# Attention stage of a three-stage kernel: the output product in two halves, with a reordered load and store queue

## The chip, the core and the metric

The program runs on one core of a Trainium2 chip. The metric is the time of one execution on the device in microseconds (us). Before the change the median of three runs is 898.57 us (898.33 to 898.73).

A core has TensorE (matrix products and transposes, into PSUM), VectorE, ScalarE and GpSimd, and SyncE, which in this kernel only issues transfers (DMAs) between DRAM and SBUF. Each engine works through its own list of instructions in order, and an engine waits for another by semaphores that are written into the lists. In the rows the engines are PE, DVE, ACT, POOL and SP.

## What is computed

Three stages, one behind the other, all in float32. The first is attention in 32 heads of 576 positions with a block-wise causal mask; the second a gated feed-forward layer; the third a mixture of eight experts, of which each token takes one.

```python
def _attn_ref(q, k, v):            # q, k, v: (4, 8, 576, 64)
    scores = scale * np.matmul(q, k.transpose(0, 1, 3, 2))
    mask = block_i >= block_j      # blocks of 64 positions
    scores = np.where(mask, scores, -1000000000.0)
    scores = scores - np.max(scores, axis=-1, keepdims=True)
    attn = np.exp(scores)
    attn = attn / (np.sum(attn, axis=-1, keepdims=True) + 1e-09)
    return np.matmul(attn, v)

x = attention output as (2304, 512)
x = (1 / (1 + np.exp(-(x @ w_gate)))) * (x @ w_val) @ w_out      # d_ff 1536
out = mixture of experts of x
```

## The kernel before

**Attention, pair by pair.** The heads go in 16 pairs (g = 0 to 15; p = g mod 4, b = g div 4), since two heads of 64 dimensions fill 128 partitions. A pair is worked through in nine steps i = 0 to 8, from the widest block row (576 columns of scores) to the narrowest (64). In a step, TensorE makes scores in PSUM (`scores`, L1455; step 0 makes the widest row, step 1 the next two, steps 3, 5 and 7 two each), VectorE takes the negated row maximum (`nmax`, L1068), ScalarE the exponential with its row sum (`prob`, L869), and TensorE turns tiles of the probabilities (`turn`, L1466), which VectorE and ScalarE copy out of PSUM into `pt` (L383, by the tables `OUT_V` and `OUT_A`). The work is staggered: the turns of the last four rows of a pair fall into steps 0 to 3 of the next one, and the product with V (`pv`, L1493) is made in steps 4 and 6 of the next pair, into `bank[3]`, columns 0 to 319 in one half and 320 to 575 in the other. TensorE's scores of step 3 need the first exponential of their own pair (`exp_done`), those of step 5 the third; before it turns the last tile it waits for ScalarE's and VectorE's copies of the two tiles before the previous ones (`out_by`).

**Dividing by the row sums.** In step 1, VectorE adds 1e-9 to the sums of the pair before (`recips`, L1031) and takes their reciprocals (L1037 to L1039, semaphore `rinv_done`). SyncE stores them in DRAM (`rinv_store`, L533) and loads them back spread over the partitions into `rwide` (`rwide_load`, two transfers, L541), of which there is only one. At step 8, behind its last maximum, VectorE multiplies the product by `rwide` into `xo` (`o_out`, L1047, one instruction for each half, the 320 columns first) and raises `xo_done`. SyncE stores `xo` to `xt_dram` (`o_store`, L528). TensorE may write `bank[3]` again, and SyncE load `rwide` again, only once `xo_done` has been raised for the pair before.

**SyncE's list** in its round of pair g, L555 to L589: K and Q of pair g (L566, L567, once all scores of pair g-2 are made), store and spread load of the reciprocals of pair g-2, a w1 load (L548) in every even round and in the last, or in round 13 the whole first group of x (`xload`, L597), then V (L580, L583, once the product with V of pair g-2 is done), and last the store of `xo` of pair g-2. Round g runs while the engines work on pair g-1.

**GpSimd's list** in its round of pair g: it scales K by 1/8 (L747) once K and Q have landed; then in some rounds it splits weights into a float32r part and a rest (`w1_split`: cast L727, subtraction L730), or x in round 13 (`x_split`, L735, L739). The subtraction waits for the reciprocals of pair g-1 (`rinv_done`), the cast doesn't. For the second stage, TensorE's first product (`up(0, 0)`) needs the splits of x and of all eight w1 loads.

The second stage starts with TensorE at about 177 us, beside the last turns of pair 15, and the third follows.

## Time and profile before

| | |
|---|---|
| median of three runs | 898.57 us |
| the profiled execution's own time | 897.07 us |
| its span, first to last instruction | 895.4 us |
| granted TensorE clock, mean | 0.998 |
| TensorE matmuls busy | 880.5 us (98%) |
| VectorE busy | 472.2 us (53%) |
| ScalarE busy | 304.3 us (34%) |
| GpSimd busy | 201.9 us (23%) |
| widest maxima, L1068 | 16, about 0.75 us each |
| products into xo, L1047 | 32 (16 pairs of halves), 1.25 us a pair |

One execution was profiled. Times of instructions are counted from the span's start. A line of a timeline has the start, the time from the first start to the last end of the merged instructions, the engine, the line of the kernel, what is written and read with its size, and in brackets how long the engine sat idle before it and who released it. The ends of matmuls are modelled, and TensorE counts as busy also where it is short of its peak; transfers are seen from issue to landing.

### The profile page before, as it was taken

The numbers are of one execution on the slowest core, as the hardware profiler recorded it, in microseconds if no ns is written. First come the engines' busy times: TensorE is split into PE (matmuls) and PEld (weight loads), VectorE is DVE, ScalarE is ACT, GpSimd is POOL, SyncE is SP. The second block draws the span as 40 slices with busy tenths as digits, with TensorE's granted clock in tenths as the row PEclk, the third lists the DMA queues.
The fourth block names the chain that finished last, engine by engine and source line by source line (L and its number), as shares of the span: only waits on it lengthen the run. The fifth ranks groups of instructions, "written<-read, shape, count | busy, mean of one in ns | idle before, by whom it ended". The sixth has DMA issues, their size and how long they took to land.

```text
span 895.4 us, 15054 instructions
## 1 busy us (share of the span) xinstructions
PE 880.5 (98%) x5216; PEld 730.4 (82%) x5217; DVE 472.2 (53%) x1094; ACT 304.3 (34%) x702; POOL 201.9 (23%) x233
## 2 busy tenths in 40 slices
PE   8999999999999999999999999999999999999996
PEld 5555555599999999999999999999888888888885
DVE  6777777743244335435325443656575636483253
ACT  5555555543231121112112112224333424362141
POOL 2222234312121212212111211122122222232221
PEclk9999999999999999999999999999999999999999
DMA  4554555554320010002002000033355535474111
GB/s 119 165 156 152 154 161 173 153 161 138 130 72 1 1 41 31 1 1 72 1 1 71 1 1 1 36 110 115 118 164 200 168 112 195 140 236 145 47 37 40
DMA packets 49410, 85.42 MB, mean 95 GB/s; under 512 B 9527, under 2 KB 21815, under 8 KB 49216
## 3 DMA queue, kind: packets, MB, share of 16 engines
q1 hardware_dynamic: 43440, 69.30, 24.5%
q0 software_dynamic: 3360, 10.50, 3.8%
q10 hardware_dynamic: 2544, 4.75, 1.4%
q8 instruction: 39, 0.64, 0.3%
q14 instruction: 27, 0.22, 0.1%
HBM read 70.28 MB, written 14.78 MB: 95 GB/s over the span
## 4 chain that ended last, share of the span: by engine, by line
PE 88%; DVE 6%; DMA 2%; issue 2%; ACT 1%; POOLq 1%; POOL 0%; SPq 0%; DVEq 0%
PE bank L1519 20%; PE bank L1521 20%; PE bank L1520 20%; PE bank L1493 5%; PE bank L1466 4%; PE bank L1690 4%; PE bank L1691 4%; PE bank L1695 4%; PE bank L1455 3%; DVE nmax L1068 2%; DVE xo L1047 2%; PE bank L1674 2%; ACT prob L869 1%; PE bank L1637 1%; DMA yg<-y_scratch,gcol 1%
## 5 line engine op out<-in xcount | busy, mean ns | idle before, releaser
L1519 PE MATMUL bank<-xh,w1h 128*128 128x384 f32 x576 | 194.0, 337 | 0.0
L1521 PE MATMUL bank<-xh,w1l 128*128 128x384 f32 x576 | 193.1, 335 | 0.0
L1520 PE MATMUL bank<-xl,w1h 128*128 128x384 f32 x576 | 192.8, 335 | 0.0
L768 POOL TENSOR_TENSOR hl<-hraw,hh 128x384 fp32r<-128x384 f32 x72 | 85.3, 1185 | 370.2 <-ACT hh L895 370.2
L1255 DVE TENSOR_TENSOR hraw<-hraw,bank 128x384 f32<-128x384 f32 x72 | 39.9, 554 | 224.1 <-ACT hraw L940 224.0
L940 ACT ACTIVATE hraw<-bank 128x384 f32<-128x384 f32 x72 | 35.4, 492 | 229.9 <-PE bank L1521 229.9
L1519 PEld LDWEIGHTS bank<-xh,w1h 128*128 128x128 f32 x576 | 108.2, 188 | 2.4
L1520 PEld LDWEIGHTS bank<-xl,w1h 128*128 128x128 f32 x576 | 108.2, 188 | 2.2
L1521 PEld LDWEIGHTS bank<-xh,w1l 128*128 128x128 f32 x576 | 108.1, 188 | 0.0
L869 ACT ACTIVATE prob<-bank,nmax 128x576 f32<-128x576 f32 (+2 forms) x144 | 75.5, 526 | 72.5 <-DVE nmax L1068 69.7
L1521 PE MATMUL bank<-woh,hl 128*128 128x512 f32 x216 | 85.3, 395 | 0.0
L1520 PE MATMUL bank<-wol,hh 128*128 128x512 f32 x216 | 85.1, 394 | 0.0
L1519 PE MATMUL bank<-woh,hh 128*128 128x512 f32 x216 | 84.3, 390 | 0.0
L1466 PEld LDWEIGHTS bank<-ident,prob 128*128 128x128 f32 x400 | 43.3, 140 | 38.7 <-issue 30.2
L383 DVE COPY pt<-bank 128x512 f32<-128x512 f32 (+1 forms) x96 | 52.8, 550 | 39.9 <-PE bank L1466 39.9
L1455 PE MATMUL bank<-kt,qt 64*64 64x64 f32 (+7 forms) x640 | 68.7, 424 | 3.2 <-ACT prob L869 1.3
L1068 DVE TENSOR_REDUCE nmax<-bank 128x1 f32<-128x576 f32 (+2 forms) x144 | 66.6, 481 | 3.6 <-PE bank L1455 3.1
L1466 PE MATMUL bank<-ident,prob 128*128 128x128 f32 x400 | 66.0, 286 | 2.1 <-DVE pt L383 1.2
L895 ACT CAST hh<-hraw 128x384 fp32r<-128x384 f32 x72 | 37.0, 514 | 86.4 <-PE bank L1521 79.6
L1519 PE MATMUL bank<-w1h,ygh 128*128 128x512 f32 x160 | 64.1, 401 | 0.6 <-DVE ygl L1237 0.6
L1521 PE MATMUL bank<-w1h,ygl 128*128 128x512 f32 x160 | 62.4, 390 | 0.0
L1520 PE MATMUL bank<-w1l,ygh 128*128 128x512 f32 x160 | 62.4, 390 | 0.0
(211 smaller groups left out, 1329.7 us busy)
## 6 DMA issues: line engine op xcount, KB each, us to landing
stage<-in_we SPq DMA_DIRECT2D x56, 512.0 KB, 3.9
kt<-in_kT SPq DMA_DIRECT2D x16, 288.0 KB, 3.3
rwide<-rinv_scratch SPq DMA_DIRECT2D x32, 144.0 KB, 2.9
xt_scratch<-xo SPq DMA_DIRECT2D x16, 288.0 KB, 2.1
xraw<-xt_scratch SPq DMA_DIRECT2D x6, 768.0 KB, 4.8
y_scratch<-yrow ACTq DMA_DIRECT2D x6, 768.0 KB, 5.3
qt<-in_qT SPq DMA_DIRECT2D x15, 288.0 KB, 3.5
vt<-in_v SPq DMA_DIRECT2D x16, 256.0 KB, 2.8
```

The source lines that it names most:

```text
L383: copy(bass.AP(tensor=rows.tensor, offset=rows.offset + PT_STEP * t0 + first + BLK * i, ap=[rows.ap[0], [PT_STEP, t1 - t0], [to_next, 2], ...
L768: pool.tensor_tensor(hl[:, f % 2, :], hraw[:, f % 2, :], hh[:, f % 2, :].bitcast(F32), ALU.subtract).then_inc(h_low, 1)
L869: act.activation(prob[:, prob_at[i]:prob_at[i] + width(i)], scores_at(p, i), ACT.Exp, bias=nmax[:, i:i + 1], accum_out=rsum[:, p % 2, ORDE ...
L895: act.copy(hh[:, f % 2, :], hraw[:, f % 2, :]).then_inc(h_high, 1)
L1068: dve.tensor_reduce(nmax[:, i:i + 1], scores_at(p, i), AX.X, ALU.max, negate=True).then_inc(nmax_done, 1)
L1255: dve.tensor_tensor(hraw[:, f % 2, :], hraw[:, f % 2, :], val_ps, ALU.mult).then_inc(hraw_done, 1)
L1455: last = pe.matmul(sc[64 * hh:64 * hh + 64, a:e], qt[p % 2][d, BLK * i:BLK * i + BLK], kt[p % 2][d, a:e], start=True, stop=True, skip_grou ...
L1466: last = pe.transpose(pT_psum(u)[:, (t - t0) * P:(t - t0 + 1) * P], prob[:, prob_at[j] + P * t:prob_at[j] + P * t + P], ident[:])
L1493: last = pe.matmul(oT_at(h, a, e), vt[p % 2][0:K, j, 64 * h:64 * h + 64], pt[p % 2][0:K, PT_STEP * j + S * h + a:PT_STEP * j + S * h + e], ...
L1519: pe.matmul(out_, wh, ah, start=first, stop=False, skip_group_check=True)
L1520: pe.matmul(out_, wh, al, start=False, stop=False, skip_group_check=True)
L1521: return pe.matmul(out_, wl, ah, start=False, stop=last, skip_group_check=True)
```

## The change

`o_out` becomes `o_half`: the first half still stands at step 8 behind the last maximum of the pair, the second moves into step 0 of the next pair, behind its widest maximum and the copy of that step, and raises `xo_done` there. In SyncE's round g the store of `xo` no longer stands at the end but behind the spread load of the reciprocals, and is that of pair g-3; so K and Q of the next round directly follow V. The load of x's first group is made in two halves (two of four chunks each), in rounds 11 and 13, each with a semaphore of its own, and GpSimd splits it in the same halves. GpSimd's splits wait for the reciprocals ahead of the cast instead of between cast and subtraction. At the end of attention the two halves of pairs 14 and 15 follow each other directly as before.

```diff
         pv_done = sem("pv_done")
         xo_done = sem("xo_done")
         xo_stored = [sem(f"xo_stored{i}") for i in range(2)]
+        x0_loaded = [sem(f"x0_loaded{i}") for i in range(2)]
         x_loaded = sem("x_loaded")
         x_high = sem("x_high")
         x_low = sem("x_low")
...
 
         OUT_V = {0: (1, 5), 1: (1, 7), 3: (0, 0), 4: (0, 1), 5: (0, 2), 6: (0, 3)}
         OUT_A = {0: (1, 6), 2: (1, 8), 3: (0, 0), 8: (0, 4)}
-        X_PAIR = NPAIR - 3
+        X_HALVES = {NPAIR - 5: 0, NPAIR - 3: 1}
 
         PV_STEP = {4: [0], 6: [1, 2, 3, 4]}
         RSUM_STEP, O_STEP = 1, 8
+        assert O_STEP == NB - 1
 
         def evac_pT(copy, p, j, u, t0, t1, done):
 
...
         @block.sync
         def _(sp):
 
-            def o_store(b, p):
-
-                sp.wait_ge(xo_done, b * PPB + p + 1)
+            def o_store(g):
+                b, p = divmod(g, PPB)
+                sp.wait_ge(xo_done, g + 1)
                 sp.dma_start(xt_dram[p, :, bass.ds(b * S, S)], xo[p % 2][:]).then_inc(xo_stored[p % 2], 16)
 
             def rinv_store(g, par):
...
                 if not early:
                     rinv_store(g - 2, p % 2)
                     rwide_load(g - 2, p % 2)
+                    if g >= 3:
+                        o_store(g - 3)
                     if p % 2 == 0:
                         w1_load(g // 2 - 1)
                     elif g == NPAIR - 1:
                         w1_load(2 * C - 1)
-                    elif g == X_PAIR:
-                        xload(0, PPB)
+                    elif g in X_HALVES:
+                        x_half_load(X_HALVES[g])
                     sp.wait_ge(pv_done, g - 1)
                 if isinstance(g, int) and g == 0:
                     sp.wait_ge(qk_loaded[0], 32)
...
                 sp.dma_start(vt[p % 2][0:64, KT_N - 1, :],
                              v[bass.ds(g, 1), (KT_N - 1) * P:S, :].rearrange("a k d -> k (a d)")
                              ).then_inc(v_loaded[p % 2], 16)
-                if p >= 2:
-                    o_store(b, p - 2)
-                elif not (isinstance(b, int) and b == 0):
-                    o_store(b - 1, p + 2)
+
+            def x_half_load(h):
+                for i in range(2):
+                    sp.wait_ge(xo_stored[i], 16 * PPB // 2)
+                cs = slice(C // 2 * h, C // 2 * (h + 1))
+                sp.dma_start(xraw[:, cs, :], xt_dram[cs, :, 0:GT].rearrange("c p n -> p c n")).then_inc(x0_loaded[h], 16)
 
             def xload(G, pairs_stored):
                 for i in range(2):
...
                 for p in range(PPB):
                     pair(b, p)
             sp.dma_start(wr_sb[:], wr.rearrange("(c p) e -> p c e", p=P)).then_inc(wr_loaded, 16)
+            o_store(NPAIR - 3)
             rinv_store(NPAIR - 2, 0)
             rwide_load(NPAIR - 2, 0)
 
...
 
             wo_load(0)
             wo_load(1)
-            o_store(BATCH - 1, PPB - 2)
+            o_store(NPAIR - 2)
             rinv_store(NPAIR - 1, 1)
             rwide_load(NPAIR - 1, 1)
             sp.wait_ge(pv_done, NPAIR)
             for k in range(2, FC):
                 if k == 4:
-                    o_store(BATCH - 1, PPB - 1)
+                    o_store(NPAIR - 1)
                 sp.wait_ge(wo_high, k - 1)
                 sp.wait_ge(wo_low, k - 1)
                 wo_load(k)
...
                 pool.wait_ge(w1_loaded, 16 * (k + 1))
                 raw = w1raw[:, 0:FL].rearrange("p (f n) -> p f n", n=P)
                 h, lo = w1h[:, 0:FE, k, :], w1l[:, 0:FE, k, :]
+                pool.wait_ge(rinv_done, g)
                 pool.tensor_copy(h, raw).then_inc(w1_high, 1)
                 pool.wait_ge(w1_high, k + 1)
+                pool.tensor_tensor(lo, raw, h.bitcast(F32), ALU.subtract).then_inc(w1_low, 1)
+
+            def x_split(half, g):
+                cs = slice(C // 2 * half, C // 2 * (half + 1))
+                raw, h, lo = (x[:, cs, :].rearrange("p c n -> p (c n)") for x in (xraw, xh, xl))
+                pool.wait_ge(x0_loaded[half], 16)
                 pool.wait_ge(rinv_done, g)
-                pool.tensor_tensor(lo, raw, h.bitcast(F32), ALU.subtract).then_inc(w1_low, 1)
-
-            def x_split():
-
-                pool.wait_ge(x_loaded, 16)
-                pool.tensor_copy(xh[:].rearrange("p c n -> p (c n)"), xraw[:].rearrange("p c n -> p (c n)")
-                                 ).then_inc(x_high, C)
-                pool.wait_ge(x_high, C)
-                pool.wait_ge(rinv_done, X_PAIR)
-                pool.tensor_tensor(xl[:].rearrange("p c n -> p (c n)"), xraw[:].rearrange("p c n -> p (c n)"),
-                                   xh[:].rearrange("p c n -> p (c n)").bitcast(F32), ALU.subtract
-                                   ).then_inc(x_low, C)
+                pool.tensor_copy(h, raw).then_inc(x_high, C // 2)
+                pool.wait_ge(x_high, C // 2 * (half + 1))
+                pool.tensor_tensor(lo, raw, h.bitcast(F32), ALU.subtract).then_inc(x_low, C // 2)
 
             def pair(b, p):
                 g = b * PPB + p
...
                     w1_split(2 * b, g)
                 elif p == 0 and not (isinstance(b, int) and b == 0):
                     w1_split(2 * b - 1, g)
-                elif p == 1 and isinstance(b, int) and b == BATCH - 1:
-                    x_split()
+                elif g in X_HALVES:
+                    x_split(X_HALVES[g], g)
 
             for b in range(BATCH - 1):
                 for p in range(PPB):
...
                 pair(BATCH - 1, p)
 
             def xhigh(G, cs):
-                act.wait_ge(x_loaded, 16 * (G + 1))
+                act.wait_ge(x_loaded, 16 * G)
                 for c in cs:
                     act.copy(xh[:, c, :], xraw[:, c, :]).then_inc(x_high, 1)
 
...
                 dve.reciprocal(to[0:64, :, 0], of[64:128, :, 0])
                 dve.reciprocal(to[64:128, :, 0], of[0:64, :, 0]).then_inc(rinv_done, 1)
 
-            def o_out(g, par):
+            def o_half(g, par, half):
                 dve.wait_ge(pv_done, g + 1)
-                dve.wait_ge(rwide_loaded, 32 * (g + 1))
-                if not (isinstance(g, int) and g < 2):
-                    dve.wait_ge(xo_stored[par], 8 * (g - par))
-                for half, i0, i1 in ((0, 0, 5), (1, 5, NB)):
-                    last = dve.tensor_tensor(
-                        xo[par][:, BLK * i0:BLK * i1].rearrange("p (i q) -> p i q", q=BLK),
-                        rwide[:, :, i0:i1].rearrange("p q i -> p i q"),
-                        bank[3][:, half, 0:BLK * (i1 - i0)].rearrange("p (i q) -> p i q", q=BLK), ALU.mult)
-                last.then_inc(xo_done, 1)
+                if half == 0:
+                    dve.wait_ge(rwide_loaded, 32 * (g + 1))
+                    if not (isinstance(g, int) and g < 2):
+                        dve.wait_ge(xo_stored[par], 8 * (g - par))
+                i0, i1 = ((0, 5), (5, NB))[half]
+                last = dve.tensor_tensor(
+                    xo[par][:, BLK * i0:BLK * i1].rearrange("p (i q) -> p i q", q=BLK),
+                    rwide[:, :, i0:i1].rearrange("p q i -> p i q"),
+                    bank[3][:, half, 0:BLK * (i1 - i0)].rearrange("p (i q) -> p i q", q=BLK), ALU.mult)
+                if half:
+                    last.then_inc(xo_done, 1)
 
             def after_unit(g, p, j):
 
...
                     if i in OUT_V and not (start and OUT_V[i][0]):
                         back, j = OUT_V[i]
                         after_unit(g - back, p - back, j)
+                    if i == 0 and not (isinstance(g, int) and g < 2):
+                        o_half(g - 2, p % 2, 1)
                     if i == RSUM_STEP and not start:
                         recips(g - 1, (p - 1) % 2)
                     if i == O_STEP and not start:
-                        o_out(g - 1, (p - 1) % 2)
+                        o_half(g - 1, (p - 1) % 2, 0)
 
             for b in range(BATCH - 1):
                 for p in range(PPB):
...
                     dve.tensor_tensor(xl[:, c, :], xraw[:, c, :], xh[:, c, :].bitcast(F32), ALU.subtract
                                       ).then_inc(x_low, 1)
 
+            o_half(NPAIR - 2, 0, 1)
             after_unit(NPAIR - 1, 1, 5)
             recips(NPAIR - 1, 1)
             after_unit(NPAIR - 1, 1, 7)
...
                     dve.wait_ge(sig_done, n + 1)
                     dve.tensor_tensor(hraw[:, f % 2, :], hraw[:, f % 2, :], val_ps, ALU.mult).then_inc(hraw_done, 1)
                     if first and f == 1:
-                        o_out(NPAIR - 1, 1)
+                        o_half(NPAIR - 1, 1, 0)
+                        o_half(NPAIR - 1, 1, 1)
                     if first:
                         dve.wait_ge(wo_high, f + 1)
                         dve.tensor_tensor(wol[:, f, :], wo_raw(f), woh[:, f, :].bitcast(F32),
```

## Rows read from the trace of the kernel before

**Rows 1.** The windows view, behind the attention stage: length, busy time by engine, clock, DMA.

```profile
196.00:895.40 699.40, 691.01 (x3571) 620.51 (x3569) 331.64 (x744) 196.35 (x340) 147.11 (x176) 1.00 0.25 79
```

**Rows 2.** Timeline of VectorE, widest maximum of pair 2 and of pair 13.

```profile
25.45 0.74 DVE L1068 TENSOR_REDUCE nmax<-bank 128x1 f32<-128x576 f32 x1
...
146.65 0.76 DVE L1068 TENSOR_REDUCE nmax<-bank 128x1 f32<-128x576 f32 x1
```

**Rows 3.** Timeline of VectorE around the boundary from pair 11 to pair 12.

```profile
133.58 1.25 DVE L1047 TENSOR_TENSOR xo<-rwide,bank 128x320 f32<-128x320 f32 x2
134.77 0.73 DVE L1068 TENSOR_REDUCE nmax<-bank 128x1 f32<-128x576 f32 x1
135.43 0.40 DVE L383 COPY pt<-bank 128x256 f32<-128x256 f32 x1
135.76 0.67 DVE L1068 TENSOR_REDUCE nmax<-bank 128x1 f32<-128x512 f32 x1
...
136.56 0.15 DVE L1031 TENSOR_SCALAR rsum<-rsum 128x9 f32<-128x9 f32 x1
```

**Rows 4.** Timeline of ScalarE, same boundary.

```profile
135.54 0.74 ACT L869 ACTIVATE prob<-bank,nmax 128x576 f32<-128x576 f32 x1 [0.85 <-DVE nmax L1068]
...
136.52 0.70 ACT L869 ACTIVATE prob<-bank,nmax 128x512 f32<-128x512 f32 x1
...
137.58 0.27 ACT L383 COPY pt<-bank 128x128 f32<-128x128 f32 x1 [0.27 <-PE bank L1466]
138.00 0.63 ACT L869 ACTIVATE prob<-bank,nmax 128x448 f32<-128x448 f32 x1 [0.16 <-PE bank L1466]
```

**Rows 5.** Timeline of TensorE, same boundary.

```profile
133.00 1.19 PE L1455 MATMUL bank<-kt,qt 64*64 64x512 f32 x8
...
135.49 0.78 PE L1466 MATMUL bank<-ident,prob 128*128 128x128 f32 x3
136.42 0.86 PE L1455 MATMUL bank<-kt,qt 64*64 64x384 f32 x8
...
138.16 1.19 PE L1493 MATMUL bank<-pt,vt 128*64 128x320 f32 x8
139.28 0.65 PE L1455 MATMUL bank<-kt,qt 64*64 64x256 f32 x8
```

**Rows 6.** Timeline of SyncE's transfers, same boundary.

```profile
132.52 0.52 SPq L583 DMA_DIRECT2D vt<-in_v  x1
...
135.71 0.46 SPq L567 DMA_DIRECT2D qt<-in_qT  x1
137.34 0.33 SPq L533 DMA_DIRECT2D rinv_scratch<-rinv  x1
139.39 1.09 SPq L541 DMA_DIRECT2D rwide<-rinv_scratch  x2
```

**Rows 7.** Transfers of line L567, the 15 loads of Q: issue to landing.

```profile
DMA to landing us min/median/max: 3.1/3.5/4.0
```

**Rows 8.** Transfers of line L533, the 16 stores of reciprocals: issue to landing.

```profile
DMA to landing us min/median/max: 1.4/2.1/2.7
```

**Rows 9.** L541, two spread loads each: at 84.7 (w1 behind), at 139.4 (x behind).

```profile
DMA to landing us min/median/max: 2.8/3.6/4.4
...
DMA to landing us min/median/max: 2.9/4.2/5.5
```

**Rows 10.** Timeline of VectorE at the boundary to pair 13.

```profile
145.48 1.26 DVE L1047 TENSOR_TENSOR xo<-rwide,bank 128x320 f32<-128x320 f32 x2 [0.87 <-issue]
...
148.44 0.41 DVE L1031 TENSOR_SCALAR rsum<-rsum 128x9 f32<-128x9 f32 x1
```

**Rows 11.** Timeline of GpSimd, from 137 us on.

```profile
137.47 1.82 POOL L730 TENSOR_TENSOR w1l<-w1raw,w1h 128x768 fp32r<-128x768 f32 x1 [3.22 <-DVE rinv L1039]
139.29 1.65 POOL L747 TENSOR_SCALAR kt<-kt 128x576 f32<-128x576 f32 x1
147.36 1.47 POOL L735 CAST xh<-xraw 128x1536 fp32r<-128x1536 f32 x1 [6.41 <-DMA xraw<-xt_scratch]
```

## The prediction

> **What bounds the kernel now.** I read the windows first: behind 196 us TensorE is busy for 691.01 of 699.40 us [rows 1], in dense layers whose instructions the change doesn't touch. So the change acts in the attention stage alone, before about 180 us. There the timeline of VectorE gives the beat. Its widest maximum (576 columns) comes once a pair: from 25.45 [rows 2] to 134.77 [rows 3] are ten pairs, 10.93 us each; then one of 11.88 us, to 146.65 [rows 2].
>
> Around such a pair boundary the three engine timelines have to be laid side by side. The reader is to see a relay. VectorE runs without a pause: the product into xo 133.58 to 134.83, the widest maximum 134.77 to 135.50, a copy, the next maximum from 135.76 [rows 3]. (An instruction starts about 0.07 before the one ahead of it has ended; I keep that.) The scores that the widest maximum reads were finished at 134.19 (133.00 + 1.19) [rows 5]: the maximum waits for the product, not for scores. ScalarE's exponential starts at 135.54 after 0.85 idle and ends at 136.28 [rows 4]; TensorE has finished its transposes at 136.27 and starts the next scores at 136.42 [rows 5], 0.14 behind that exponential.
>
> **Part 1, the product halved.** Nothing is computed that wasn't before. The 256-column half has 4/9 of the columns, some 0.6 of the 1.25, and the two end at 134.83 [rows 3], so it starts at 134.24; in the new order the maximum starts there, 0.05 after its scores are finished, and 0.53 earlier than now. Then, all shifted by 0.53: maximum to 134.97, exponential 135.01 to 135.75, scores from 135.89 at the earliest. TensorE must be free by then. Its three transposes start at 135.49; the third waits for VectorE's copy, now 135.43 to 135.83 [rows 3], then 134.90 to 135.30, so they run through and are done by about 135.9. Scores: gain 0.5.
>
> What is late next? The second half goes behind that copy: 135.24 to 135.83, and the second maximum starts at 135.76, exactly as now: VectorE had no idle time here, its work is only reordered. So the second exponential, now 136.52, moves by 0.05 at most, to 136.47, and ends at 137.17. ScalarE's copy behind it now starts at 137.58, because it waits 0.27 for a transpose of TensorE [rows 4]. That transpose, the one behind the scores, comes 0.5 earlier, so the copy is released by the exponential, at 137.17 instead: 0.41 earlier. Its tile is the last that TensorE turns before the product with V, now 138.16 [rows 5]. That goes to 137.75. **The gain here is 0.41**; the remaining 0.1 is TensorE's wait for ScalarE. Next scores: now 139.28 [rows 5], then 138.87; they need the third exponential, whose maximum is not earlier (ends 138.63 [rows 4], plus 0.14: 138.77). This just doesn't bind, by 0.1. From there to the next boundary TensorE leads and VectorE and ScalarE follow it, so the whole pair moves by 0.41. The added waits of the second half are for things long done; behind it stand the second maximum, the copy and the reciprocals, at their old times. The boundaries at which the half is parted from its first are those behind pairs 1 to 14: 14 x 0.41 = **5.7 us**. Behind pair 15's maxima both halves are adjacent as now: nothing.
>
> **Part 2, the queue of SyncE.** Now it issues V (132.52), then waits for xo (134.83), stores it, and only then issues K and Q (135.71), the store of the reciprocals at 137.34 and its spread load into rwide at 139.39 [rows 6]. With the store of xo moved behind the spread load, K and Q go out at once behind V: Q at about 133.55, and with the 3.5 median [rows 7] it lands at 137.1, before the reciprocals' store instead of during it. That store takes 1.4 at best and 2.1 at the median [rows 8]; alone in the queues I give it 1.4: landed at 138.75, the two spread loads at 138.75 and 139.25, 0.64 earlier than now. They are needed by the first half of the next product, in the new beat at 133.58 + 10.93 - 0.41 = 144.10. The second may thus take 4.85. Behind it there now go the store of xo and, in every other pair, the w1 load. With w1 alone behind it, it took 4.4, with the whole x load 5.5 [rows 9]. Both ends: 0 (it takes 4.4) and a stall of 0.65 (5.5) in each such pair, seven with w1 and two with a half of x. I take 0 for the seven with w1, nearer to its own row (4.4, and the store is smaller than the x load's excess over w1), and 0.2 for each of the two with x, nearer to the x load's: -0.4 in all.
>
> **Part 3, x in two halves.** The one long period is that of the x load: the spread load took 5.5, the product waited 0.87 [rows 10], and the add ahead of the reciprocals took 0.41 instead of 0.15. Gone: 11.88 - 10.93 = 0.95 us. Two halves follow in pairs 10 and 12, each as large as a w1 load (counted above). GpSimd does the same splits in two pieces.
>
> **Part 4, GpSimd waits for the reciprocals before its cast** rather than between cast and subtraction. Its cast moves and is covered: the cast (some 0.75, half of the 1.47 of twice the columns) and the subtraction (1.82) from 137.3 end at 139.9, the scaling of K behind them (1.65) at 141.6 [rows 11], and K is needed one period after 133.00 [rows 5], at 143.5. What it removes: the cast that ran from 147.36 to 148.83 [rows 11] held up a VectorE add until 148.85 [rows 10]. Worth nothing elsewhere, since elsewhere the add takes 0.15.
>
> **Sum:** 5.7 + 0.95 - 0.4 = 6.3 us. The profiled execution had a span of 895.4 and a time of 897.07, so 1.7 outside the span, and lies 1.5 below the median of 898.57. The same saving from each: span 889.1, median **892.3**.
>
> **Rivals.**
>
> *A: K scaling lands on the reciprocals.* Q lands 2 us earlier, and GpSimd scales K when it does. In the pairs where GpSimd has no split ahead (3, 5, 7 and 9; in 1 the load doesn't move, in 11 and 13 the x halves stand ahead), the scaling starts at Q's landing. If that is before the add at 136.56 [rows 3], the add waits for its end, as in [rows 10, 11]: 1.65 from, say, 136.5 gives 138.15, 1.45 late; then the third maximum and exponential are 1.45 late and the next scores start at 140.2 instead of 138.87. That takes 1.35 in 4 pairs: 5.4 us, so 897.7. Against it: Q from 133.55 with the shortest landing of 15, 3.1 [rows 7], comes at 136.65, just too late to do harm; the reciprocals themselves I take as unhurt. The Trainium skill (SBUF — State Buffer, "Who interferes with whom") says that a VectorE instruction in a two-port mode, for which it names copy, cast and tensor_scalar, and a GpSimd instruction exclude each other for their whole length, whichever starts first. The trace agrees for the one add that met a cast, 0.41 instead of 0.15; reciprocals are not among the named. If they were hurt too, this rival would hold more often than I give it.
>
> *B: the spread load becomes the bound (the slower end).* If with store and w1 behind it the second spread load takes 6.0 instead of at most 4.85, the product stalls 1.15 at nine boundaries: 10.4 against 6.7 gained, so 902.3. It is slower than before from 5.6 on, just above the 5.5 that the x load caused with more bytes behind it. For it: two transfers now follow. Against it: it is issued 0.64 earlier, and K and Q are out of the way.
>
> *C: less is gained.* The third exponential or the second maximum slips by 0.1 to 0.3 for a reason that the rows don't show (the margin is only 0.1), or the spread load takes about 5.3 in the nine pairs. Half of the gain is left: about 895.3.
>
> *D: more.* Without ScalarE's late copy the gain is the whole 0.53, and the spread load never stalls: 14 x 0.53 + 0.95 = 8.4, so 890.2.
>
> **How the numbers follow.** Forecast (890.9 to 894) 0.60; C 0.17; D 0.07; A 0.09; B 0.07. Range: D's end to C with part of A: 890.2 to 896.5; what lies outside is A, B and a little of D, under 0.2. A measurement of this kernel tells about 0.2%, 1.8 us, from no change: faster (below 896.8) = forecast + C + D + a little of A: 0.85; same 0.09, most of A; slower 0.06, most of B.
>
> **What would show it.** In the profile of the changed kernel the widest maximum should start 0.66 after the first half starts, and the second half stand behind the 256-column copy; the period should be 10.52 and all 15 alike; TensorE's scores should start within 0.1 of its transposes' end; K and Q should be issued at once behind V, and the reciprocals' store land in 1.4 to 1.6. Idle time of VectorE before the first half would mean B (or part of C); an add of over 1 us ahead of the reciprocals would mean A; ScalarE idle before the third exponential, with TensorE waiting for it, would mean C. If the period didn't shorten although the maximum came earlier, my chain through the second exponential is wrong.

## Result and profile after

The changed kernel takes 892.06 us (median of four runs, 891.85 to 892.26), the kernel before, run beside it, 898.45 (896.87 to 898.73). The ratio is 0.9932, with a 95% interval of 0.9915 to 0.995: 6.4 us less, well over the 0.2% (1.8 us) that a measurement of this kernel can tell. The forecast was 892.3, range 890.2 to 896.5. The profiled execution took 892.18, with a span of 890.5.

First VectorE around the boundary that [rows 3] shows of before (columns: start, duration, engine, line, operation, what is written and read):

```profile
129.06 0.71 DVE L1053 TENSOR_TENSOR xo<-rwide,bank 128x320 f32<-128x320 f32 x1
129.71 0.76 DVE L1075 TENSOR_REDUCE nmax<-bank 128x1 f32<-128x576 f32 x1
130.39 0.41 DVE L385 COPY pt<-bank 128x256 f32<-128x256 f32 x1
130.72 0.61 DVE L1053 TENSOR_TENSOR xo<-rwide,bank 128x256 f32<-128x256 f32 x1
131.24 0.69 DVE L1075 TENSOR_REDUCE nmax<-bank 128x1 f32<-128x512 f32 x1
...
140.23 0.76 DVE L1075 TENSOR_REDUCE nmax<-bank 128x1 f32<-128x576 f32 x1
```

The widest maximum now starts 0.65 behind the first product (before: 1.19), the second half stands behind the copy, and the second maximum starts 2.18 behind the first product, exactly as before (135.76 less 133.58). The period from 129.71 to 140.23 is 10.52, the next 10.56. From the first widest maximum to the last it is 155.76 us instead of 162.55: 6.79 saved. These are 15 periods; the first of them has no work of an earlier pair in it and is 8.5 us in both kernels, so the saving lies in the other 14.

ScalarE and TensorE in the same stretch, to be laid beside [rows 4] and [rows 5]:

```profile
130.50 0.74 ACT L874 ACTIVATE prob<-bank,nmax 128x576 f32<-128x576 f32 x1 [0.34 <-DVE nmax L1075]
131.96 0.69 ACT L874 ACTIVATE prob<-bank,nmax 128x512 f32<-128x512 f32 x1
132.64 0.25 ACT L385 COPY pt<-bank 128x128 f32<-128x128 f32 x1
133.50 0.63 ACT L874 ACTIVATE prob<-bank,nmax 128x448 f32<-128x448 f32 x1 [0.61 <-DVE nmax L1075]
```

```profile
128.47 1.19 PE L1466 MATMUL bank<-kt,qt 64*64 64x512 f32 x8
...
131.44 0.86 PE L1466 MATMUL bank<-kt,qt 64*64 64x384 f32 x8
...
133.21 1.19 PE L1504 MATMUL bank<-pt,vt 128*64 128x320 f32 x8
...
134.33 0.65 PE L1466 MATMUL bank<-kt,qt 64*64 64x256 f32 x8
```

The reader is to see that ScalarE's copy at 132.64 has no idle time before it any more, where [rows 4] had 0.27 behind TensorE. The page says the same of the whole run. Its first part, then its fourth, the chain of work that ended last, where before had PE 88% and DVE 6%:

```profile
PE 878.6 (99%) x5216; PEld 731.1 (82%) x5217; DVE 472.3 (53%) x1094; ACT 305.7 (34%) x702; POOL 201.5 (23%) x235
...
PE 95%; DVE 2%; DMA 1%; issue 1%; POOLq 1%; ACT 0%; POOL 0%; DVEq 0%
```

Between the first and the last widest maximum TensorE is busy for 153.84 of 155.76 us, where before it was busy for 157.35 of 162.55, with as good as the same number of matmuls (1418 and 1421 in the trace). So about half of the saving is idle time of TensorE, and the other half is time in which it counted as busy without more work being done. Last, SyncE in the same period (issues; compare [rows 6]), and the landings of its stores of the reciprocals (L535), spread loads (L543) and Q (L569):

```profile
128.55 0.58 SPq L568 DMA_DIRECT2D kt<-in_kT  x1
129.18 0.43 SPq L569 DMA_DIRECT2D qt<-in_qT  x1
132.84 0.33 SPq L535 DMA_DIRECT2D rinv_scratch<-rinv  x1
134.26 1.63 SPq L543 DMA_DIRECT2D rwide<-rinv_scratch  x2
135.93 0.58 SPq L530 DMA_DIRECT2D xt_scratch<-xo  x1
...
DMA to landing us min/median/max: 1.4/1.6/2.6
...
DMA to landing us min/median/max: 2.8/3.0/4.7
...
DMA to landing us min/median/max: 3.0/4.0/4.5
```

Q is issued 3.7 us ahead of the reciprocals' store instead of 1.6, and the store lands in 1.6 at the median instead of 2.1 [rows 8].

### The profile page after: what moved, and what is told of

It is laid out like the page before. It is cut to its first block, busy times and chain, and to the rows that moved or that the text cites. A ratio compares the mean times of both kernels' runs of the same rounds, so it can differ in the third digit from the quotient of the medians.

```text
span 890.5 us, 15060 instructions
## 1 busy us (share of the span) xinstructions
PE 878.6 (99%) x5216; PEld 731.1 (82%) x5217; DVE 472.3 (53%) x1094; ACT 305.7 (34%) x702; POOL 201.5 (23%) x235
## 3 DMA queue, kind: packets, MB, share of 16 engines
q0 software_dynamic: 3360, 10.50, 3.9%
## 4 chain that ended last, share of the span: by engine, by line
PE 95%; DVE 2%; DMA 1%; issue 1%; POOLq 1%; ACT 0%; POOL 0%; DVEq 0%
PE bank L1530 21%; PE bank L1532 21%; PE bank L1531 20%; PE bank L1466 7%; PE bank L1477 6%; PE bank L1504 6%; PE bank L1701 4%; PE bank L1702 4%; PE bank L1706 4%; PE bank L1685 2%; PE bank L1648 1%; DMA yg<-y_scratch,gcol 1%; DMA out<-orow,scol 1%; PE bank L1440 0%; PE bank L1596 0%
## 5 line engine op out<-in xcount | busy, mean ns | idle before, releaser
L1466 PE MATMUL bank<-kt,qt 64*64 64x512 f32 (+7 forms) x640 | 68.4, 423 | 1.3 <-ACT prob L874 1.2
L1477 PE MATMUL bank<-ident,prob 128*128 128x128 f32 x400 | 63.7, 285 | 0.7 <-DVE pt L385 0.6
```

The costliest lines, as they stand in the source:

```text
L1466: last = pe.matmul(sc[64 * hh:64 * hh + 64, a:e], qt[p % 2][d, BLK * i:BLK * i + BLK], kt[p % 2][d, a:e], start=True, stop=True, skip_grou ...
L1477: last = pe.transpose(pT_psum(u)[:, (t - t0) * P:(t - t0 + 1) * P], prob[:, prob_at[j] + P * t:prob_at[j] + P * t + P], ident[:])
```

## The experiments

A period below is the distance from one widest maximum to the next. Runs e1 to e4 share one set of runs of the kernel before (median 898.26), e5 to e8 another (898.18); e9 and e10 stand beside one run of 896.59, e11 beside one of 897.87.

### e1: the halved product alone

The kernel before, in which only the product's second half moves; SyncE, x and GpSimd stay.

```diff
                     if i in OUT_V and not (start and OUT_V[i][0]):
                         back, j = OUT_V[i]
                         after_unit(g - back, p - back, j)
+                    if i == 0 and not (isinstance(g, int) and g < 2):
+                        o_half(g - 2, p % 2, 1)
                     if i == RSUM_STEP and not start:
                         recips(g - 1, (p - 1) % 2)
                     if i == O_STEP and not start:
-                        o_out(g - 1, (p - 1) % 2)
+                        o_half(g - 1, (p - 1) % 2, 0)
```

> The kernel before with only the product halved; order of the queue, load of x and waits of GpSimd as before. Times against 898.45 us before and 892.06 us after. My theory (halving gains 0.41 at each of 14 boundaries, but only if the spread load lands in time): the second half raises its semaphore 1.0 us later than the whole product did (135.83 instead of 134.83 in the rows of before), so the store of xo, K and Q are issued 1.0 later, the store of the reciprocals (2.0 to 2.7 us in that order) is not faster, and the spread load, 4.4 us with a w1 load behind it, lands up to 0.8 after the product wants it. So the boundaries without w1 gain 0.41 and those with w1 gain nothing: about -2.5 us, 896.0 us, with idle time of VectorE ahead of the first half in every second pair. Rival (the queue's order adds nothing): all 14 boundaries gain, -5.7 us, 892.8 us, pairs of 10.52 us throughout but for the one of the x load.

Measured: 905.34 us (902.84 to 905.76), ratio 1.0075 (1.0051 to 1.0099). The half of the change that carries the gain makes the kernel slower by itself. SyncE and the product that waits, in this kernel's trace:

```profile
119.11 0.33 SPq L528 DMA_DIRECT2D xt_scratch<-xo  x1
119.48 0.43 SPq L566 DMA_DIRECT2D kt<-in_kT  x1
119.96 0.56 SPq L567 DMA_DIRECT2D qt<-in_qT  x1
120.59 0.39 SPq L533 DMA_DIRECT2D rinv_scratch<-rinv  x1
...
124.57 1.09 SPq L541 DMA_DIRECT2D rwide<-rinv_scratch  x2
...
128.59 0.72 DVE L1048 TENSOR_TENSOR xo<-rwide,bank 128x320 f32<-128x320 f32 x1 [1.18 <-issue]
...
DMA to landing us min/median/max: 1.4/3.3/5.1
...
DMA to landing us min/median/max: 2.8/3.1/4.3
```

`xo_done` is raised 1.0 us later in the pair (the second half ends at 118.47 + 0.62, which is 2.26 behind the first half's start at 116.83, where [rows 3] have 1.25). The old list waits for it before it issues K and Q, so they go out directly ahead of the reciprocals' store, 0.63 from Q to store instead of 1.63 [rows 6]. Here the store takes 4 us (the next issue behind it is at 124.57), and over all pairs 3.3 at the median, up to 5.1. The spread loads themselves are as fast as ever (3.1). Periods are 10.50 where the chain isn't late and 10.7 to 12.6 elsewhere. VectorE sits idle for 0.33 to 1.97 ahead of twelve products, 13.0 in all, and that is most of the 14.4 by which the 14 full periods are longer than those of the changed kernel (161.7 against 147.3). My expectation was wrong, and on the wrong side of the kernel before: 2.5 us faster was said, 7 slower measured. Its reason was right (the spread load comes too late), but I had taken the reciprocals' store at 2.0 to 2.7, and expected only the pairs with a w1 load to be late.

### e2: the queue's order alone

The kernel before, in which only SyncE stores `xo` of pair g-3 behind the spread load.

```diff
                     rwide_load(g - 2, p % 2)
+                    if g >= 3:
+                        o_store(g - 3)
...
-                if p >= 2:
-                    o_store(b, p - 2)
-                elif not (isinstance(b, int) and b == 0):
-                    o_store(b - 1, p + 2)
```

> The kernel before with only SyncE's order changed (K and Q directly behind V, the store of xo behind the spread load); product whole, x in one load. My theory: the product isn't held up by the queue in 13 of 14 boundaries, so the pairs stay at 10.93 us; the reciprocals' store lands in 1.4 to 1.7 us instead of 2.1, and only the stall of 0.87 us ahead of the product in the pair of the x load can change, by -0.6 to 0: 898.1 us. Rival (the queue's order is itself a part of the gain): more than 2 us faster, 896.4 us or less. Second rival (K is scaled on top of the add ahead of the reciprocals): pairs of up to 12.3 us, 903 us.

Measured: 897.19 us (896.05 to 898.96, ten runs), ratio 0.9997 (0.9985 to 1.0009). As expected, no difference that the times can tell: the periods stay at 10.92 to 11.01, since nothing waited for the transfers in them. The period with x is 11.29 instead of 11.88. The product no longer stalls there; what is left is the add held up by the cast of the whole x (GpSimd, then VectorE):

```profile
147.25 1.46 POOL L734 CAST xh<-xraw 128x1536 fp32r<-128x1536 f32 x1 [6.10 <-DMA xraw<-xt_scratch]
147.72 1.02 DVE L1030 TENSOR_SCALAR rsum<-rsum 128x9 f32<-128x9 f32 x1
```

### e3: everything but the halving

The changed kernel with both halves of the product at step 8.

```diff
                     if i == O_STEP and not start:
                         o_half(g - 1, (p - 1) % 2, 0)
+                        o_half(g - 1, (p - 1) % 2, 1)
```

(The call in step 0 is left out.)

> The changed kernel with the product whole again at step 8; queue, x in halves and GpSimd's waits as changed. My theory: only the stall of the x load is gone: -0.95 us, 897.5 us, all 15 pairs of 10.93 us. Rival (the halves are not what shortens the pair): 892 to 895 us.

Measured: 897.16 us (895.78 to 899.5, ten runs), ratio 0.9996 (0.9981 to 1.0011); all 14 full periods are 10.92 to 11.01, 0.91 less in all than before. That is part 3's 0.95, seen in the trace but within what the times can tell. So of 6.79 us saved, 0.91 is x, and 5.9 come from the halving, which e1 shows to need the new queue.

### e4: x in one load again

The changed kernel, with x loaded and split whole in round 13.

```diff
-        X_HALVES = {NPAIR - 5: 0, NPAIR - 3: 1}
+        X_PAIR = NPAIR - 3
...
-                cs = slice(C // 2 * h, C // 2 * (h + 1))
-                sp.dma_start(xraw[:, cs, :], xt_dram[cs, :, 0:GT].rearrange("c p n -> p c n")).then_inc(x0_loaded[h], 16)
+                sp.dma_start(xraw[:], xt_dram[:, :, 0:GT].rearrange("c p n -> p c n")).then_inc(x0_loaded[0], 16)
```

> The changed kernel with x's first group in one load and one split again (round 13). My theory: behind the second spread load of that round there are then the store of xo and 768 KB; it takes 5.5 us as before or, if the store adds to it, some 6.2, against 4.85 that the beat allows: a stall of 0.65 to 1.35 us in one pair, 893.1 us, the other pairs at 10.52 us. Rival (x in halves brings nothing once K and Q are out of the way): no stall, 892.1 us.

Measured: 893.44 us (892.12 to 894.85, five runs), ratio 0.9955 (0.9937 to 0.9973). The size is as expected, the cause is not. The spread load landed in time. What is late is GpSimd (its lines, then VectorE's):

```profile
144.62 1.47 POOL L742 CAST xh<-xraw 128x1536 fp32r<-128x1536 f32 x1 [6.20 <-DVE rinv L1042]
146.24 3.45 POOL L744 TENSOR_TENSOR xl<-xraw,xh 128x1536 fp32r<-128x1536 f32 x1 [0.15 <-POOL xh L742]
149.66 1.65 POOL L750 TENSOR_SCALAR kt<-kt 128x576 f32<-128x576 f32 x1
...
152.63 0.76 DVE L1073 TENSOR_REDUCE nmax<-bank 128x1 f32<-128x576 f32 x1 [0.69 <-PE bank L1464]
```

Cast and subtraction of twice the columns, both behind the reciprocals, push the scaling of K to 151.31; TensorE starts the scores then, 0.70 late, and the widest maximum waits 0.69. That period is 11.27. (Two others are 10.69 and 10.86, in part by a product that waited 0.26; see e7.) In this kernel x has to be halved for the split's sake, not for the transfer's.

### e5: GpSimd's casts no longer wait for the reciprocals

The changed kernel with the order of waits as before, in `w1_split` (shown) and `x_split`.

```diff
-                pool.wait_ge(rinv_done, g)
                 pool.tensor_copy(h, raw).then_inc(w1_high, 1)
                 pool.wait_ge(w1_high, k + 1)
+                pool.wait_ge(rinv_done, g)
```

> The changed kernel with GpSimd's casts released by their load alone again, the subtraction by the reciprocals. My theory: nothing changes, 892.1 us, since the loads land and are cast over 1 us before the add ahead of the reciprocals (w1 at the latest 88.29 and 129.96 us, the add at 89.97 and 132.03); at most one add, that of 163.66, meets the cast of the last w1 load, 0.8 us at one boundary. Rival (the moved wait is a part of the gain): casts meet adds in three pairs or more, adds of over 0.4 us in the timeline, 1 us or more lost.

Measured in one run: 891.63 us, span 889.9. Every add takes 0.155 to 0.171, and a single product stalls, by 0.21. As expected, part 4 is worth nothing here, where x comes in halves; what it can be worth with the whole x is e2's add of 1.02, in a period that is 0.36 longer.

### e6: the second half one place later

The changed kernel with the second half behind the second maximum.

```diff
+                    if i == 1 and not (isinstance(g, int) and g < 2):
+                        o_half(g - 2, p % 2, 1)
                     if i in OUT_V and not (start and OUT_V[i][0]):
                         back, j = OUT_V[i]
                         after_unit(g - back, p - back, j)
-                    if i == 0 and not (isinstance(g, int) and g < 2):
-                        o_half(g - 2, p % 2, 1)
```

> The changed kernel with the second half one place further back, behind the second maximum. The scores of the second maximum are only finished 0.3 to 0.4 us after VectorE is free for it, a time which the second half now fills. My theory: VectorE waits there, and maximum three and its exponential come 0.3 to 0.35 later; the scores behind them have 0.06 us of room, so 0.3 of the 0.41 are lost at each boundary: pairs of 10.8 us, +4 us, 896 us. Rival (VectorE has room, and the second exponential, now earlier by 0.15, takes away TensorE's last wait of 0.1): pairs of 10.42 us, 890.7 us.

Measured: 897.08 us (895.46 to 898.15, ten runs), ratio 0.9988 (0.9976 to 0.9999); most periods are 10.85 (the 14 full ones, 10.50 to 11.15, add up to 4.2 more than in the changed kernel). VectorE, ScalarE and TensorE, each a line or two:

```profile
101.98 0.69 DVE L1075 TENSOR_REDUCE nmax<-bank 128x1 f32<-128x512 f32 x1 [0.28 <-PE bank L1466]
102.59 0.61 DVE L1053 TENSOR_TENSOR xo<-rwide,bank 128x256 f32<-128x256 f32 x1
...
104.77 0.64 ACT L874 ACTIVATE prob<-bank,nmax 128x448 f32<-128x448 f32 x1 [1.01 <-DVE nmax L1075]
...
105.55 0.65 PE L1466 MATMUL bank<-kt,qt 64*64 64x256 f32 x8
```

The second maximum, moved forward, only gets to wait 0.28 for its scores; the second half then delays the third maximum, and with it the third exponential and TensorE. At the place that the change chose, the half fills the time in which VectorE would have waited. One place further costs 0.33 of the 0.41 in most pairs.

### e7: the store of xo ahead of the reciprocals' store

The changed kernel, with K and Q still first but the large store between them and the small one.

```diff
                     sp.dma_start(qt[p % 2][:], qkv_at(qT, g)).then_inc(qk_loaded[p % 2], 16)
+                if g >= 3:
+                    o_store(g - 3)
                 if not early:
                     rinv_store(g - 2, p % 2)
                     rwide_load(g - 2, p % 2)
-                    if g >= 3:
-                        o_store(g - 3)
```

> The changed kernel with the store of xo between the load of Q and the store of the reciprocals, instead of behind the spread load. The store waits for the second half (131.3 us in the rows of after), the reciprocals follow at 132.8. My theory: what gave the spread load its time is that K and Q are out of the way (the reciprocals' store took 2.7 to 5.1 us directly behind them, 1.4 to 2.2 in the changed kernel), and a store of xo issued 1.5 us ahead costs it under 1 us more; the spread load then has fewer bytes behind it. 892 to 894 us, pairs of 10.5 us, single stalls of up to 0.5. Rival (the place of the store is what counts): the reciprocals' store takes over 3 us, VectorE idles ahead of the first half in most pairs, 897 us or more.

Measured: 892.06 us (890.8 to 893.4, four runs), ratio 0.994 (0.9922 to 0.9958). The landings of the reciprocals' store:

```profile
DMA to landing us min/median/max: 1.4/1.6/3.2
```

One period is 11.09, with 0.38 idle ahead of the product, the others 10.50 to 10.52. That stall isn't particular to e7: among the profiles with the new queue, those of the changed kernel and of e10 have none, those of e4 to e9 and e11 each have one to three products that wait 0.15 to 1.00, and single stores of the reciprocals take up to 3.6. So the new queue has little room, and that the changed kernel's own profile shows no such wait is in part luck.

So the place of the store of `xo` is not what matters. Taking K and Q out of the wait for `xo_done`, ahead of the reciprocals' store by some microseconds, is the enabling edit. e1 against e7 shows it, though e1 also lacks the halving of x, which e4 prices at 1.4 us, and the moved wait of GpSimd, which e5 prices at nothing.

### e8 to e10: what holds VectorE's add

Rival A rested on one row, an add that met a cast. In these three kernels GpSimd does one instruction more in four of the pairs (periods 3, 5, 7, 9), on tiles that nothing else uses then, started in e8 and e9 0.56 ahead of the add. (In e9 to e11 SyncE's load of x also waits until the four are done.) In e8 it is four times a tensor_scalar of 512 columns:

```diff
+            def extra_op(g):
+                pool.wait_ge(extra, g // 2 - 1)
+                pool.wait_ge(xo_done, g - 2)
+                pool.tensor_scalar(yg[:, 0:512], yg[:, 0:512], SCALE, None, ALU.mult).then_inc(extra, 1)
```

> The changed kernel with one more GpSimd operation, a tensor_scalar over 512 columns of an unused tile, in pairs 3, 5, 7 and 9, released by the second half of the product, so that it starts 0.7 us ahead of the add in front of the reciprocals and runs over its start. My theory: in these pairs the add ends with the GpSimd operation, about 0.8 late, and the pair gets about 0.75 longer (the third exponential has 0.06 of room): +3 us, 895 us. Rival (the pair has room for a late add): adds long, pairs 10.5 us, 892 us. Second rival (a 9-column add doesn't need what GpSimd holds): adds of 0.17 us.

Measured in one run: 892.7 us. The adds take 0.157 to 0.170 though they fall into the middle of the instruction as the profile shows it, so my first theory was wrong. (One of the four periods is 10.94, with a product that waited 0.35.)

```profile
38.17 1.49 POOL L737 TENSOR_SCALAR yg<-yg 128x512 f32<-128x512 f32 x1 [4.70 <-DVE xo L1065]
...
38.74 0.16 DVE L1048 TENSOR_SCALAR rsum<-rsum 128x9 f32<-128x9 f32 x1
```

In e9 the four are of 1536 columns and of four kinds:

```diff
+                if g == 4:
+                    ins = pool.tensor_copy(h, raw)
+                elif g == 6:
+                    ins = pool.tensor_copy(raw, raw)
+                elif g == 8:
+                    ins = pool.tensor_tensor(lo, raw, h.bitcast(F32), ALU.subtract)
+                else:
+                    ins = pool.tensor_scalar(raw, raw, SCALE, None, ALU.mult)
```

> The changed kernel with one more GpSimd operation over 1536 columns in each of the pairs 3, 5, 7 and 9, released by the second half, so that it is under way when the add ahead of the reciprocals comes up 0.7 us later: in pair 3 a cast to float32r (1.5 us), in 5 a copy in float32, in 7 a subtraction of two tiles (3.4), in 9 a product with a constant. The add took 0.17 beside a tensor_scalar in the run before this one, and 0.41, 0.73 and 1.02 us beside casts in three others, each time ending with the cast. Theory 1 (only a cast or copy holds VectorE's add): the adds of pairs 3 and perhaps 5 take 0.8 to 0.9 us and those pairs 11.3 us, those of 7 and 9 take 0.17. Theory 2 (every GpSimd operation that reads and writes SBUF holds it): all four late, up to 2.8 us in pair 7, and the tensor_scalar of the earlier run was a chance. Theory 3 (only the float32r output counts): pairs 3 and 7.

Measured in one run: 905.64 us. GpSimd's lines for the cast and the tensor_scalar, each with VectorE's add behind it:

```profile
38.95 1.46 POOL L740 CAST xh<-xraw 128x1536 fp32r<-128x1536 f32 x1 [4.67 <-DVE xo L1074]
...
39.52 0.92 DVE L1057 TENSOR_SCALAR rsum<-rsum 128x9 f32<-128x9 f32 x1
...
108.02 4.09 POOL L746 TENSOR_SCALAR xraw<-xraw 128x1536 f32<-128x1536 f32 x1 [4.71 <-DVE xo L1074]
...
108.57 3.56 DVE L1057 TENSOR_SCALAR rsum<-rsum 128x9 f32<-128x9 f32 x1
```

Every kind held the add (0.92, 0.92, 2.90 and 3.56), and it ended 0.03 behind GpSimd's instruction. The two delays of 0.75 cost 0.94 and 0.71 in their periods (11.46, in which a product also waited 0.16, and 11.23). The delay of 2.7 costs 4.3 (14.83), and that of 3.4 costs 6.1 (16.63), because TensorE comes out of the idle time at its lower level, 1.2 GHz: from 109.2 to 116.0 it is busy for 3.52 of 6.80 us, at a mean granted clock of 0.80, and from 116.0 to 118.0 busy throughout at 0.50. The four periods together are 12.1 longer; another 1.1 is a product that waited for its spread load in period 1, before the first of the four instructions.

e10 has the same four, waiting for `rsum1_done` instead, so that they start beside the first reciprocal:

```diff
-                pool.wait_ge(xo_done, g - 2)
+                pool.wait_ge(rsum1_done, g - 1)
```

> As the run before, but the GpSimd operation is released by the add itself, so that it starts beside the first reciprocal and runs over the other two and the third and fourth maximum. My theory (the reciprocals and maxima don't need what a cast takes from the add): reciprocals of 0.18 us, maxima of 0.62 and 0.55, all pairs 10.52 us but where K is scaled late behind the subtraction of 3.4 us. Rival: reciprocals that end with the cast, about 1.3 us late, in pair 3 and perhaps 5.

Measured in one run: 893.58 us. Reciprocals take 0.18 to 0.19 everywhere, the adds of these pairs 0.16 to 0.17, and those periods are 10.52 to 10.65. Reciprocals and maxima run beside any of the four at their usual length; only the add is held.

### e11: sizes

The tensor_scalar again, at the place of e8, in place on 512, 576 and 1024 columns of x's tile and on e8's own.

```diff
+                tile = {4: raw[:, 0:512], 6: raw[:, 0:576], 8: yg[:, 0:512], 10: raw[:, 0:1024]}[g]
+                pool.tensor_scalar(tile, tile, SCALE, None, ALU.mult).then_inc(extra, 1)
```

> As the run with four kinds on the add, but all four GpSimd operations are products with a constant, in place, in float32: in pair 3 over 512 columns of x's tile, in 5 over 576 (K's size), in 7 over 512 columns of the other tile used first, in 9 over 1024. It settles why the add was held by 1536 columns (3.56 us) and not by 512 of the other tile (0.17). Theory S (size: the operation lets go of what the add needs well before the end that the profile shows, or a short one is over by then): 3 and 7 at 0.17, 9 held, 5 in between. Theory T (the tile): 7 at 0.17, the other three held, the add ending with the GpSimd operation. Either way the price of a held add: about the delay of the add, less 0.06, on the pair.

Measured in one run: 894.17 us. GpSimd and VectorE for 576 and 1024 columns, then the scaling of K in the first round, which meets an add by itself:

```profile
60.78 1.65 POOL L742 TENSOR_SCALAR xraw<-xraw 128x576 f32<-128x576 f32 x1 [4.71 <-DVE xo L1069]
...
61.33 0.17 DVE L1052 TENSOR_SCALAR rsum<-rsum 128x9 f32<-128x9 f32 x1
...
102.85 2.77 POOL L742 TENSOR_SCALAR xraw<-xraw 128x1024 f32<-128x1024 f32 x1 [4.71 <-DVE xo L1069]
...
103.40 0.51 DVE L1052 TENSOR_SCALAR rsum<-rsum 128x9 f32<-128x9 f32 x1
...
17.62 1.65 POOL L768 TENSOR_SCALAR kt<-kt 128x576 f32<-128x576 f32 x1 [5.54 <-DMA qt<-in_qT]
...
18.77 0.52 DVE L1052 TENSOR_SCALAR rsum<-rsum 128x9 f32<-128x9 f32 x1
```

Both adds of 512 columns (either tile) and that of 576 pass. That of 1024 is held until 103.91, 1.7 before GpSimd is done; that of K, which comes 1.15 into an instruction of 576 columns, until its end. So the tile doesn't decide, and whether an add is held depends on the size of GpSimd's instruction and on the point of it at which the add comes, not only on the kind. What in the instruction makes the difference stays open, the more so as the profile gives GpSimd's spans only roughly.

## Why the prediction was right, point by point

**Part 1, the chain through ScalarE.** Each step came within 0.02 of its place, counted from the first product: the maximum at 0.65 (said: 0.66), the second at 2.18 (as before), the second exponential at 2.90 (2.89), ScalarE's copy at 3.58 (3.59), the product with V at 4.15 (4.17), the next scores at 5.27 (5.29). The copy is released by the exponential, not by the turn, which is where 0.41 rather than 0.53 comes from. The margin of the third exponential was said to be 0.1; it ends at 134.13, plus 0.14 is 134.27, and the scores start at 134.33: 0.06. e6 supports that this chain is the one that counts: 0.33 put into it came back as 0.33 in most periods, 4.2 us over the 14. Part 1 as a whole is 5.9 instead of 5.7.

**Part 2, the queue.** The mechanism stood: the store landed at 1.6, the spread loads within the 4.85 allowed (4.7 at most), and in this profile VectorE was idle ahead of no first half (in others with this queue it was, see e7). Two terms were mis-sized. Q takes 4.0 at the median instead of the 3.5 that I took from [rows 7]. So it is still under way when the store is issued 3.7 us behind it, not landed as I had it; the store took 1.6 instead of 1.4 and no product waited, so the error cost nothing. And the 0.4 that I charged to the halves of x is nothing: the spread loads with a half of x behind them took 3.2 and 3.6 at most, and the periods in which their products fall are 10.52. It is those with a w1 load behind them, for which I had taken 4.4, that come near the limit of 4.85: three of them took 4.6 or 4.7. One of the three (issued at about 145.5, landed at 150.1) ends where the product of the period of 10.56 starts, 0.04 late. There are eight of these, not seven: the last w1 load stands in round 15. What I had not seen is that part 1 can't do without this part: I treated it as a gain of 0.64 in a transfer that had room, and asked what the transfers behind the spread load cost. The question that decides is what the old queue would do with the later `xo_done`, and e1 answers it: lose 7 us.

**Part 3, x.** 0.95 said, 0.91 measured (e3). The reason given, the spread load of 5.5, holds in the kernel before; in the new order the whole x would have cost about as much (e4: 11.27 less 10.52 is 0.75 in its period) by another route, GpSimd's splits ahead of the scaling of K.

**Part 4, GpSimd's wait.** Said to be worth nothing beyond the add that met the cast of the whole x; e5 agrees.

**The sum.** 6.3 said; 6.79 between the widest maxima. The span of the profiled execution is 890.5, not 889.1, and the reason lies outside attention. In the third stage, up to the choice of the experts, TensorE is 6.9 us ahead of before (635.79 against 642.72 for the same instruction), and from there to its turns of `yg` it loses 2.1 (673.47 less 635.79 is 37.68, against 35.58). Windows of the two kernels at that instruction (columns: window, length, busy time of PE, PEld, DVE, ACT and POOL with their instructions, granted clock, share and GB/s of the DMA engines):

```profile
635.00:638.90 3.90, 3.90 (x13) 3.03 (x11) 2.22 (x12) 0.82 (x2) 0.00 (x0) 0.56 0.05 0
```

```profile
642.00:645.90 3.90, 3.90 (x19) 3.23 (x18) 3.20 (x20) 0.82 (x2) 0.00 (x0) 1.00 0.04 0
```

In the changed kernel TensorE does 13 matmuls in this window, in the one before 19 at the full level of 2.4 GHz. For some 3.4 us of it the granted clock was at the lower level, 1.2 GHz, with matmuls 0.43 apart instead of 0.23. It fell about a microsecond behind a stretch (630.0 to 634.4) of 16 turns of 128 columns and 24 matmuls of 8 columns:

```profile
633.49 1.04 PE L1596 MATMUL bank<-wr_sb,yT 128*128 128x8 f32 x8
...
673.47 0.66 PE L1648 MATMUL bank<-ident,yg 128*128 128x128 f32 x4 [0.90 <-DMA yg<-y_scratch,gcol]
```

From 635.79 on the lower level cost 1.4 us: the matmul at 638.96 starts 3.17 behind the one at 635.79, and the same two were 1.75 apart before (642.72 and 644.47). Most of the rest is in the second line: TensorE waits 0.90 for the gathered `yg`, where before it waited 0.26. The fall of the clock isn't the change's doing: the same stretch was followed by the lower level in the profiles of e1, e3, e4, e6, e9 and e10 and not in those of before, e2, e5, e7, e8 and e11, whatever was changed. e7's profile without it has a span of 889.1.

That the median came within 0.3 of the forecast is in part luck. Attention gave 0.5 more than the sum, mostly through the 0.4 charged to x, the two profiled executions differ by only 4.9, and single executions of the kernel before scatter by 1.9, so an agreement of this size says little. What bears the prediction out is the places of the chain in part 1.

**The rivals.** A didn't occur: GpSimd scales K at 101.83, 1.3 behind the add at 100.48, since Q is issued 0.12 behind the first product and lands in 4.0. Its mechanism is real (e9, 3.56 for an add of 0.17; e11, 0.52 beside a scaling of K), but its price was taken at the worst: an add that comes 0.55 into an instruction of 576 columns isn't held (e11). The Trainium skill (SBUF — State Buffer, "Who interferes with whom") has a VectorE instruction in a two-port mode and a GpSimd instruction exclude each other for the whole of the one that started first. e9 agrees with it; e8 and e11 don't, as adds of 0.16 and 0.17 pass in the middle of GpSimd's 1.49 and 1.65, and there the measurement decides, as far as GpSimd's rough spans let it. B didn't occur with the new queue. With the old one it did, as e1, and there the point where the kernel becomes slower was passed by the reciprocals' store, not by the spread load that I had watched. C and D had no place: neither a slip nor the whole 0.53.

## What to carry to other kernels

When a step on the path is put off, follow what its semaphore lets go, and move that out of the way first: here half of a product was free to wait, but the loads queued behind its completion were not, and the halving takes 5 us off the time with them moved (e3 against the changed kernel) and adds 7 without (e1). A gain in a relay of engines is to be followed to the next meeting point, where the smaller of the gains counts (0.41 of 0.53), and a piece of work that must go somewhere belongs exactly into the wait that its predecessor's advance opens; one place further cost four fifths of the gain. After it TensorE bounds attention almost alone (busy for all of the 10.52 us of a period), so that further work on VectorE's order has little to find: an estimate is 0.17 us a pair at this boundary, since the six turns ahead of the product with V take 1.04 and the six at 138.19 take 0.87.

## What the runs showed of the hardware

- A store of 4.5 KB in the same queue takes 1.6 us at the median, up to 2.6, when the two loads of 288 KB ahead of it have had 3.7 us to land (after), and 3.3 at the median, up to 5.1, when it is issued 0.6 us behind them (e1).
- VectorE's add of 9 columns is held by a GpSimd cast, copy, subtraction or tensor_scalar of 1536 columns to the end of that instruction (e9: 0.92 to 3.56 instead of 0.17). Reciprocals (0.18) and maxima (1.09 for two of 448 and 384 columns, as elsewhere) aren't held by any of them (e10). Tensor_scalars of 512 and 576 columns let an add pass 0.55 us behind their start (e8, e11), one of 576 held it 1.15 behind its start, one of 1024 held it for 0.51, 1.7 short of its end. The reason is open, and GpSimd's spans are rough in the profile.
- A stall of VectorE of 3.4 us cost 6.1 us, as TensorE's granted clock was at its lower level when work came back (e9, 0.50 from 116 to 118 us with the engine busy throughout).
- The granted clock fell to its lower level for some 3.4 us behind a stretch of 16 turns and 24 matmuls of 8 columns in seven of the thirteen profiles and not in the other six, in kernels whose mean is 0.991 to 0.999. In the changed kernel's profile this cost at least 1.4 us.
